# A mixture-of-experts router that searches thresholds: the count matrix turned over, experts on the rows and cuts on the columns

## The reference

```python
logits = x @ w_gate
order = np.argsort(-logits.flatten())
for idx in order:
    tok, e = (int(idx) // E, int(idx) % E)
    if assigned[tok] >= 0 or counts[e] >= cap:
        continue
    assigned[tok] = e
    counts[e] += 1
...
    h = np.maximum(x[mask] @ w1[e], 0.0)
    out[mask] = h @ w2[e]
```

## Time and profile before

| | us |
|---|---|
| median of 3 executions | 882.04 |
| all three | 881.2, 883.65, 882.04 |
| profiled execution | 881.2 |
| its span (first to last instruction) | 879.5 |
| TensorE busy | 798.7 (91%) |
| VectorE busy | 607.4 (69%) |
| ScalarE busy | 352.5 (40%) |
| GpSimd busy | 267.7 (30%) |

### The profile page before, as it was taken

The page is one execution under the profiler, slowest core; times in us unless marked ns, Lnnn a source line. Parts: engine busy times, 40 slices in busy tenths (PEclk is TensorE's granted clock), DMA queues, the critical chain, the costliest instruction groups (busy, mean ns, idle before and its releaser), DMA issues.

```text
span 879.5 us, 17361 instructions
## 1 busy us (share of the span) xinstructions
PE 798.7 (91%) x6272; PEld 765.5 (87%) x6272; DVE 607.4 (69%) x1104; ACT 352.5 (40%) x765; POOL 267.7 (30%) x310
## 2 busy tenths in 40 slices
PE   5999999210899999999999999999999999999996
PEld 4999999200899999999999999999999999999995
DVE  7999997588667766766875677667668756873210
ACT  3777777111323523342343234224423443353332
POOL 3443443061003411430343034114402430252133
PEclk9999999655899999999999999999999999999998
DMA  7566662223202300220131013002201210130000
GB/s 286 194 216 215 214 213 97 71 96 102 69 1 72 99 27 32 73 92 0 48 98 51 0 60 110 27 8 83 97 9 48 91 58 0 48 122 28 1 1 28
DMA packets 22406, 70.01 MB, mean 80 GB/s; under 512 B 3040, under 2 KB 9312, under 8 KB 22368
## 3 DMA queue, kind: packets, MB, share of 16 engines
q1 hardware_dynamic: 19296, 60.06, 19.8%
q0 software_dynamic: 3072, 9.44, 3.3%
HBM read 60.05 MB, written 9.44 MB: 79 GB/s over the span
## 4 chain that ended last, share of the span: by engine, by line
issue 45%; POOL 16%; PE 14%; DVE 5%; POOLq 1%; ACT 0%; DVEq 0%; ACTq 0%
PE ps L925 13%; POOL act_lo L581 11%; POOL out L593 2%; POOL rows L565 2%; DVE at_q L683 2%; DVE cuts L680 1%; POOL this_ids L576 1%; DVE at_q L772 0%; POOLq L580 0%; POOLq L560 0%; PE ps L888 0%; POOLq L589 0%; POOLq L562 0%; POOLq L591 0%; DVE low L697 0%
## 5 line engine op out<-in xcount | busy, mean ns | idle before, releaser
L581 POOL TENSOR_TENSOR act_lo<-gate,act_hi 128x384 fp32r<-128x384 f32 x128 | 130.3, 1021 | 405.3 <-ACT act_hi L639 405.1
L634 ACT ACTIVATE gate<-ps,three 128x384 f32<-128x384 f32 x128 | 74.3, 581 | 237.3 <-PE ps L925 227.9
L925 PE MATMUL ps<-yT_hi,w_in_hi 128*128 128x384 f32 x384 | 132.8, 346 | 1.7 <-DVE yT_lo L842 1.7
L925 PE MATMUL ps<-w_out_hi,act_hi 128*128 128x384 f32 x384 | 130.2, 339 | 2.2 <-POOL act_lo L581 1.9
L925 PE MATMUL ps<-yT_lo,w_in_hi 128*128 128x384 f32 x384 | 130.0, 339 | 0.0
L925 PE MATMUL ps<-yT_hi,w_in_lo 128*128 128x384 f32 x384 | 129.7, 338 | 0.0
L925 PE MATMUL ps<-w_out_hi,act_lo 128*128 128x384 f32 x384 | 128.9, 336 | 0.0
L847 DVE SCALAR_TENSOR_TENSOR gate<-gate,ps 128x384 f32<-128x384 f32 x128 | 70.7, 552 | 83.9 <-ACT gate L634 80.5
L925 PE MATMUL ps<-w_out_lo,act_hi 128*128 128x384 f32 x384 | 128.6, 335 | 0.0
L830 DVE SCALAR_TENSOR_TENSOR act_lo<-ps,act_hi 128x384 fp32r<-128x384 f32 x64 | 35.5, 555 | 77.6 <-ACT act_hi L622 77.6
L622 ACT ACTIVATE act_hi<-ps 128x384 fp32r<-128x384 f32 x64 | 31.5, 492 | 140.8 <-PE ps L925 138.2
(11 more groups left out here) (159 smaller groups left out, 1594.7 us busy)
## 6 DMA issues: line engine op xcount, KB each, us to landing
raw<-in_w SPq DMA_DIRECT2D x48, 512.0 KB, 3.3
attn_wrk<-in_wrk SPq DMA_DIRECT2D x24, 770.5 KB, 4.8
attn_v<-in_v SPq DMA_DIRECT2D x24, 192.0 KB, 4.5
x_rows<-attn_x SPq DMA_DIRECT2D x24, 192.0 KB, 1.9
raw<-in_w_in SPq DMA_DIRECT2D x6, 512.0 KB, 5.8
raw<-in_w_out SPq DMA_DIRECT2D x6, 512.0 KB, 3.7
rows<-x_rows,gather_ids POOLq DMA_INDIRECT x24
out<-rows,scatter_ids POOLq DMA_INDIRECT x24
```

The source lines that it names most:

```text
L581: pool.tensor_tensor(act[1][:, (H1 + g) % 3, :], gate[:, g % 2, :], act[0][:, (H1 + g) % 3, :].bitcast(F32), ALU.subtract).then_inc(g_lo, 1)
L634: act_.activation(gate[:, g % 2, :], mid[g % 2], ACT.Relu, bias=three[:, 0:1]).then_inc(gate_relu, 1)
L925: last = pe.matmul(out_, w, d, start=start and n == 0, stop=stop and n == len(passes) - 1)
```

## The change

`count` swaps its operands and takes one tile at a time. `choice` of a tile is now the weight (128 rows, 8 columns) and `above` of that tile the moving operand (64 columns); 24 matmuls add into an 8 x 64 result, experts on partitions and cuts on columns. `above` is now the first 64 of each tile's 128 places in `at_q`. `find_full` is one comparison of that result with a column of needs, one need for each of the 8 partitions. `find_any` multiplies ones of 8 rows with the 8 x 64 result, so that each partition gets, for each cut, the number of full experts. `narrow` first counts the cuts with at least one (`junk` is the comparison, `passed` its sum). `update` writes the needs into a 32 x 32 block and transposes it to get them on partitions. `candidates` reads `passed` from SBUF instead of PSUM.

```diff
-        self.bound, self.need = sb("bound", [128, E]), sb("need", [128, E])
+        self.bound, self.needT = sb("bound", [128, E]), sb("needT", [32, 32])
+        self.need = sb("need", [32, 32])
...
         pool.memset(self.need[:, :], float(CAP))
+        pool.memset(self.needT[:, :], float(CAP))
...
-        above = at_q[:, 0:TILES // 2, :].rearrange("p t (h j) -> p (t h) j", h=2)
-        full_of, full = sb("full_of", [J, E], BF16), sb("full", [128, 1], BF16)
-        rest = sb("rest", [J, E])
+        above = at_q[:, :, 0:J]
+        full = sb("full", [E, J], BF16)
...
-            link(dve.memset(full[:, :], 0.0))
...
-                link(dve.tensor_tensor(rest[:, :], need[J:2 * J, :], counts[r][J:2 * J, E:2 * E], ALU.subtract))
-                link(dve.tensor_tensor(full_of[:, :], counts[r][0:J, 0:E], rest[:, :], ALU.is_ge))
-                dve.tensor_reduce(full[0:J, :], full_of[:, :], AX.X, ALU.max).then_inc(full_ready, 1)
+                dve.tensor_scalar(full[:, :], counts[r], needT[0:E, 0:1], None, ALU.is_ge).then_inc(full_ready, 1)
...
-                link(dve.scalar_tensor_tensor(low[:, r + 1:r + 2], beaten[r], steps[:, r:r + 1], low[:, r:r + 1],
+                link(dve.tensor_scalar(junk[:, :], anyone[r], 0.5, 0.0, ALU.is_ge, ALU.add, accum_out=passed[:, :]))
+                link(dve.scalar_tensor_tensor(low[:, r + 1:r + 2], passed[:, :], steps[:, r:r + 1], low[:, r:r + 1],
                                               ALU.mult, ALU.add))
...
-                link(dve.tensor_scalar(passed[:, :], beaten[ROUNDS - 1], 1.0, None, ALU.add))
+                link(dve.tensor_scalar(passed[:, :], passed[:, :], 1.0, None, ALU.add))
...
-                link(dve.tensor_scalar(need[:, :], room[:, :], 0.5, None, ALU.max))
+                link(dve.tensor_scalar(need[:, 0:E], room[0:32, :], 0.5, None, ALU.max))
+                link(dve.transpose(needT[:, :], need[:, :]))
...
-                for t in range(0, TILES, 2):
+                for t in range(TILES):
                     if t % (TILES // 2) == 0:
                         pe.wait_ge(above_ready, 2 * ROUNDS * e + 2 * (ROUNDS + r) + t // (TILES // 2) + 1)
-                    last = pe.matmul(counts[r], above[:, t:t + 2, :].rearrange("p t j -> p (t j)"),
-                                     choice[:, t:t + 2, :].rearrange("p t e -> p (t e)"),
-                                     start=(t == 0), stop=(t == TILES - 2))
+                    last = pe.matmul(counts[r], choice[:, t, :], above[:, t, :], start=(t == 0), stop=(t == TILES - 1))
...
-                pe.matmul(beaten[r], ones[:, :], full[:, :], start=True, stop=True).then_inc(any_ready, 1)
+                pe.matmul(anyone[r], ones[0:E, :], full[:, :], start=True, stop=True).then_inc(any_ready, 1)
```

More of the change, by code:

```diff
@@ L457, in experts @@
         restart, shares, slot, waiting = tables.restart, tables.shares, tables.slot, tables.waiting
-        bound, need, three, zeros = tables.bound, tables.need, tables.three, tables.zeros
+        bound, need, needT, three, zeros = tables.bound, tables.need, tables.needT, tables.three, tables.zeros
         best = sb("best", [128, TILES])
@@ L469, in experts @@
         high, passed = sb("high", [128, 1]), sb("passed", [128, 1])
-        cuts = sb("cuts", [128, J])
+        cuts, junk = sb("cuts", [128, J]), sb("junk", [128, J])
         at_q = sb("at_q", [128, TILES, 128], BF16)
-        above = at_q[:, 0:TILES // 2, :].rearrange("p t (h j) -> p (t h) j", h=2)
-        full_of, full = sb("full_of", [J, E], BF16), sb("full", [128, 1], BF16)
-        rest = sb("rest", [J, E])
+        above = at_q[:, :, 0:J]
+        full = sb("full", [E, J], BF16)
         sure, maybe = sb("sure", [128, TILES]), sb("maybe", [128, TILES])
@@ L487, in experts @@
         last_ps = [ps[:, 5 + t, 0:DM] for t in range(ET)]
-        counts = [ps[:, 5 if r < ROUNDS - 1 else 2, 0:2 * E] for r in range(ROUNDS)]
-        beaten = [ps[:, 6 if r < ROUNDS - 1 else 3, 0:1] for r in range(ROUNDS)]
+        counts = [ps[0:E, 5 if r < ROUNDS - 1 else 2, 0:J] for r in range(ROUNDS)]
+        anyone = [ps[:, 6 if r < ROUNDS - 1 else 3, 0:J] for r in range(ROUNDS)]
         within, totals = (ps[:, 2 + i, 0:2 * E * TILES] for i in range(2))
```

## The result

| | before | after |
|---|---|---|
| median of the executions of this comparison, us | 881.62 | 908.35 |
| lowest and highest | 880.16, 883.65 | 906.75, 909.86 |
| profiled execution, its span | 881.2, 879.5 | 903.22, 901.5 |
| one expert in the loop | 81.11 | 84.39 |

The ratio is 1.029, with a 95% interval of 1.027 to 1.0311. The direction was forecast, the size was not: +26.7 us against +17.9, and 908.35 lies above the range (891.0 to 907.0). The profiled execution is not among the four timed ones and faster than all of them; its trace shows 22.0 of the 26.7 us. Fourteen more executions of the same kernel on record took 904.42 to 909.1 us. Of the executions further down, one, of the kernel before with the scatter held back, took 1036.07 us at a granted clock of 0.74 and is left out of its median and ratio.

The account below looks back on a forecast made before the run. TensorE's stream in the expert loop was taken as the bound. Count steps +18.5, hidden wait -1.1 and first search +0.5 summed to +17.9 us on the 882.04 median: 899.9 us, range 891 to 907.

Parts of the forecast that it names:

- What bounds the kernel: Whole kernel: TensorE is busy 91% of the span, so every ns added to its loop stream counts, barring few waits.
- the same 0.29 tail: TensorE behind each count: the next product's weight load costs 0.29 us, whatever matmul stands ahead, unchanged by the change.
- 0 for `find_any`: find_any in the loop: its 27 ns stream hides under the 0.30 tail, cost 0; if not hidden, 0.9 us.
- if the tail grows: Sign of being wrong: the second product matmul behind a count no longer comes 0.26 us after the first.
- g: Distance between the new count's 24 matmuls: 35 ns taken, 18.5 us for 35 counts; between 29 and 41, chance 0.72.
- The rival by which the 64 columns fit under the floor: Count steps stay at 25 to 28 ns like smaller matmuls; +11.3 us at 26.7, 893.3 us; chance 0.13.
- that of loads which do not overlap: Count's weight load and matmul run in turn, g 54 ns, 915 us; chance 0.10, shared with other prices above 41.
- that of two count matmuls at once: Two narrow count matmuls share the array, 24 take 12 steps; not slower, 881.4 us or faster; chance 0.05.
- No new waits of TensorE for VectorE: Sign expected in the loop: TensorE does not come to wait for VectorE after the change.
- The hidden wait: Each expert's last round: the longer count eats TensorE's 0.15 us wait for act_lo, 7 times, -1.1 us.
- The first search: Search before the first expert, slow clock: +0.56 us a round, mostly hidden by GpSimd, leaving +0.5; ends 0 and +2.9.
- the shield: First search: GpSimd's timetable holds VectorE and hides added time; rival without it +2.9 instead of +0.5, 902 us, no chance given.

## Why the prediction was wrong, point by point

**What bounds the kernel** was right. TensorE's stream in the loop set the time, and every loss found is on it or in front of it.

**The step that failed: the passages between product and count.** The prediction read that the count starts 0.18 after the product "as if nothing had happened", that a "tail belongs to the weight load of the next product and does not depend on what stands ahead", and took "the same 0.29 tail" and 0 for `find_any`. It measured the tail on two matmuls that both filled the array, and carried it to two that do not. The four changes of part in a round cost 0.36 to 0.37, and the products' second matmuls 0.03 more: 35 x 0.40 = 14.0 us, where the sum had 0. It is the largest term of the result. The test it had named, "if the tail grows", was the right one, and the tail is what grew: 0.13 + 0.28 for 0.03 + 0.26. The rows to price it from were in the trace: L307 to L315 and L324 to L330. Its other sign, a period that grows by over 3.4 us, came too in the traces with the late signal (3.80), and not in the first (3.28).

**g was over-sized.** The prediction took the middle of 29 and 41 ns; it is 29.1, the proportional end. 35 x 0.38 = 13.3 us in place of 18.5 (at 29 the prediction's own working gave 13.7). The two misses have opposite signs, which is why the total looks closer than the working was. The rival by which the 64 columns fit under the floor (25 to 28 ns) fell too, that of loads which do not overlap (54 ns) and that of two count matmuls at once likewise. The Trainium skill (TensorE: Matmul & The Clock Gate, Back-to-back issue gap) has both: its table gives 1 to 64 columns one price of about 25 ns, which the 29.1 of this trace contradict, while its formula for full clock, N / 2.4 + 2.5, gives 29.2 for 64. The section gives the formula for a matmul by itself and calls it too low, at small N, for one that has a weight load each; the matmuls of this count have one each and still stand at 29.1. The prediction cited the table and not the formula.

**The late signal was not thought of.** The prediction asked whether VectorE would be in time for `find_any` ("`full` comes earlier than now") and counted only VectorE's own operations. That a count which ends later falls into GpSimd's scatter was nowhere in it, and its sign "No new waits of TensorE for VectorE" holds in the first profiled execution alone. 0.5 x 6 = 3.0 us.

**The hidden wait** was right in kind and too small. The prediction had -0.15 for TensorE's wait for `act_lo` behind `find_any` of the fifth round. The rows after, which answer to the earlier trace rows:

```profile
261.59 0.20 PE L893 MATMUL ps<-full,ones 8*128 8x64 bf16 x1
261.71 0.44 PE L922 MATMUL ps<-w_out_hi,act_hi 128*128 128x384 f32 x1
```

Start to start was 0.34 and is 0.13, the bare price of a way out. Without the wait it was 0.04 before, so 0.3 us of waiting are gone, not 0.15: the bracket of the earlier trace rows counts only idle time behind the matmul's modelled end. 7 x 0.3 = -2.1 us in place of -1.1. A distance of starts would have told it.

**The first search** is neither confirmed nor refuted. The time from the first count to the first product is 53.5 before, and 52.5 and 54.6 in the two traces of after; +0.5 was forecast. The 2.1 between the two lie in one place: in the fifth cut L683 takes 1.83 in the first (from 193.48, where GpSimd's next split begins at 194.51) and 3.99 in the second (from 190.67, with the split from 191.50 to 193.84). Up to the third `find_any` the search is 0.45 us longer than before in both. Of the shield, the rows show that it held in the third round: VectorE's `low` in `narrow` is held there until GpSimd's splitting ends, as `cuts` was the earlier trace rows. GpSimd and VectorE in the first trace:

```profile
183.59 2.34 POOL L76 TENSOR_TENSOR w_out_lo<-raw,w_out_hi 128x1024 fp32r<-128x1024 f32 x1 [2.52 <-ACT w_out_hi L72]
...
184.73 1.22 DVE L695 SCALAR_TENSOR_TENSOR low<-passed,steps,low 128x1 f32<-128x1 f32 x1
```

**VectorE in the loop** was right: `find_full` takes 0.27 (forecast 0.28), and no wait for VectorE's own work came up.

**The sum as it turned out**, if the four timed executions had the late signal as eight of nine traces have it: 13.3 (steps) + 14.0 (changes of part) + 3.0 (late signal) - 2.1 (fifth round) - 2.1 (product's steps) + about 0 (first search) = +26.1, for +26.7 measured. In the profiled execution, without the late signal and with a first search 1.0 shorter than before: 7 x 3.28 - 1.0 = +22.0, which is what its span shows.

## What to carry to other kernels

When a change gives a matmul fewer weight rows or columns, look at its neighbours: between it and a matmul on the whole array each passage costs as much as three of the small ones, and here the full shape, filled up with rows of zeros or with columns whose results nobody reads, was cheaper than the smaller matmul. Price a passage by the distance of starts at a place in the trace where the same kinds of shape meet, not by one where the array stays as it is. And where a step ends later, look at what the other engines begin in that moment, also those that have nothing to do with it.

## What the runs showed of the hardware

- A change between a matmul on the whole array and one on a part of it (8 or 64 columns of weights, 8 or 64 rows) costs 0.09 us in the distance of starts, in each direction, at clock 1.00 (0.06 on the way out of the `find_any` with 64 rows and one moving column). 128x48 to 128x64 costs nothing.
- With 64 moving columns in bf16 and full clock matmuls stand 29.1 ns apart with 8 columns of weights, 29.6 with 128, and 32.6 with 64.
- TensorE's signal can reach VectorE 1.7 us late while GpSimd goes through three `DMA_INDIRECT` in a row (0.96 to 1.03 us each); it then comes as the third ends, within 0.1 us. That the scatter is needed for it is shown, since moving it takes the delay away in two kernels, in both from every turn, and from `find_any` of the kernel before; that it is not enough is shown by the one trace of nine without the delay. By what path it holds a signal of TensorE's is open.
- Open: why the signals were on time in the profiled execution of after, the fastest of its kernel (903.22 us); why the product's step is 0.6 ns shorter with the change; why 64 columns of weights make slower steps than 8 or 128; and why the recurrence, the same in all these kernels, differs by 3 us between executions (the first count starts at 168.5 in two of the fourteen traces, at 170.7 to 172.1 in the others).
